# One buffer for the first weight matrix, and steps that run the second product ahead of the next first product, in an attention and two-layer mixture-of-experts kernel

## What is computed

```python
def _moe_ref(x, modality_id, w_gate, modality_bias, w1, w2):
    logits = x @ w_gate + modality_bias[modality_id]
    e_idx = np.argmax(logits, axis=1)
    ...
    for e in range(E):
        mask = e_idx == e
        if not mask.any():
            continue
        h = np.maximum(x[mask] @ w1[e], 0.0)
        out[mask] = gate_w[mask, None] * (h @ w2[e])

def _moe2_ref(x, w_gate, w_noise, noise, w1, w2):
    ...
    top2 = np.argpartition(-noisy_logits, 2, axis=1)[:, :2]
    for e in range(E):
        for k in range(2):
            mask = top2[:, k] == e
            h = np.maximum(x[mask] @ w1[e], 0.0)
            out[mask] += top2_w[mask, k, None] * (h @ w2[e])
```

## Time and profile before

| | us |
|---|---|
| median of three runs | 1207.27 |
| lowest and highest of them | 1205.92, 1213.23 |
| the profiled execution | 1211.57 |
| its span, first to last instruction | 1209.6 |

### The profile page before, as it was taken

How to read it: one execution, slowest core, us unless ns; L and a number is a source line. 1 busy time by engine, 2 the same in 40 slices (tenths; PEclk the granted TensorE clock), 3 DMA queues, 4 the chain that set the end, 5 groups by cost and what they waited for, 6 DMA issues and landing times.

```text
span 1209.6 us, 23517 instructions
## 1 busy us (share of the span) xinstructions
PE 964.3 (80%) x7285; PEld 922.6 (76%) x7286; DVE 541.7 (45%) x956; ACT 220.0 (18%) x393; POOL 361.1 (30%) x364
## 2 busy tenths in 40 slices
PE   6999998997989766627778687957887788979794
PEld 5888887997989765617778687957787778878793
DVE  8889978553223221476333324225224223343221
ACT  2223331121101011432012002102012021211010
POOL 6333341242212120054223314314313331241222
PEclk9999989898999987857899889979888888989898
DMA  6667820811101114404422414314313424221232
GB/s 245 209 219 243 290 80 18 320 41 35 48 28 55 29 41 131 156 2 157 132 35 42 139 28 131 54 29 111 72 32 77 99 39 132 34 48 28 33 46 39
DMA packets 54428, 112.70 MB, mean 93 GB/s; under 512 B 8592, under 2 KB 35472, under 8 KB 54288
## 3 DMA queue, kind: packets, MB, share of 16 engines
q1 hardware_dynamic: 34656, 71.07, 17.2%
q0 software_dynamic: 15744, 34.70, 14.5%
q10 hardware_dynamic: 3888, 4.89, 1.1%
HBM read 84.84 MB, written 25.81 MB: 91 GB/s over the span
## 4 chain that ended last, share of the span: by engine, by line
PE 73%; DVE 12%; issue 11%; DMA 2%; DVEq 1%; POOL 1%; ACT 0%; POOLq 0%; ACTq 0%
PE ps L1676 19%; PE ps L1677 18%; PE ps L1678 18%; PE ps L1588 2%; DVE hid_lo L1369 2%; PE ps L1548 2%; PE ps L1552 2%; PE ps L1517 2%; PE ps L1494 2%; PE ps L1579 1%; PE ps L1602 1%; DVE grow L890 1%; PE ps L1542 1%; PE ps L1613 1%; DVE x_lo L1364 1%
## 5 line engine op out<-in xcount | busy, mean ns | idle before, releaser
L1676 PE MATMUL ps<-x_hi,weights 128*128 128x256 f32 x984 | 300.2, 305 | 129.8 <-issue 119.2
L1676 PEld LDWEIGHTS ps<-x_hi,weights 128*128 128x128 f32 x984 | 201.4, 205 | 142.9 <-issue 136.3
L1678 PE MATMUL ps<-x_hi,weights 128*128 128x256 f32 x984 | 291.6, 296 | 1.7 <-issue 1.7
L1677 PE MATMUL ps<-x_lo,weights 128*128 128x256 f32 x984 | 291.8, 297 | 0.0
L1369 DVE SCALAR_TENSOR_TENSOR hid_lo<-ps,hid_hi 128x512 fp32r<-128x512 f32 x164 | 109.1, 685 | 347.4 <-ACT hid_hi L817 347.4
L817 ACT ACTIVATE hid_hi<-ps 128x512 fp32r<-128x512 f32 x164 | 93.7, 596 | 756.5 <-PE ps L1678 756.5
L1676 PE MATMUL ps<-weights,hid_hi 128*128 (+1 forms) x616 | 217.0, 352 | 10.4 <-issue 7.4
L669 POOL DMA_INDIRECT out_dram<-sy,dst_now x56 | 93.4, 1668 | 408.5 <-DVE sy L1382 270.7
L1677 PE MATMUL ps<-weights,hid_hi 128*128 (+1 forms) x616 | 212.2, 344 | 1.3 <-issue 1.3
L1678 PE MATMUL ps<-weights,hid_lo 128*128 (+1 forms) x616 | 211.3, 343 | 0.0
L1677 PEld LDWEIGHTS ps<-x_lo,weights 128*128 128x128 f32 x984 | 202.4, 206 | 0.0
(11 more groups left out here) (279 smaller groups left out, 1024.5 us busy)
## 6 DMA issues: line engine op xcount, KB each, us to landing
stage<-in_moe_w_dram SPq DMA_DIRECT2D x18, 1536.0 KB, 8.5
kv_in<-in_kv_T_dram SPq DMA_DIRECT2D x24, 512.0 KB, 5.7
kv_in<-in_kv_T_dram SPq DMA_DIRECT2D x24, 448.0 KB, 3.6
w_in<-in_w_T_dram SPq DMA_DIRECT2D x24, 258.5 KB, 4.1
out_dram<-zeros SPq DMA_DIRECT2D x25, 192.0 KB
x_rows<-y_tok ACTq DMA_DIRECT2D x24, 192.0 KB, 4.8
stage<-moe_rows SPq DMA_DIRECT2D x6, 768.0 KB, 4.8
stage<-in_moe_w_dram SPq DMA_DIRECT2D x2, 768.0 KB, 7.5
```

Source lines behind the costliest of these rows:

```text
L1676: pe.matmul(out_ps, hi, by_hi, start=first, stop=False)
L1677: pe.matmul(out_ps, hi, by_lo, start=False, stop=False)
L1678: return pe.matmul(out_ps, lo, by_hi, start=False, stop=final)
```

## The change

- `weights` has six parts instead of eight: one buffer for w1's two parts, two buffers for w2's. A tile `room` keeps the addresses of what follows.
- w1 of the next run is split in the last slot of a run (`w1_now`), once all four `up` of that slot are done; w2 of the next run is split in the first slot (`w2_now`). The loads of w1 and w2 wait for their own splits.
- A step on TensorE is now the whole second product of slot s (with a turn in its middle), then all four `up` of slot s+1, then a turn. There is one copy of it.
- The main loop's body holds two steps instead of four.
- On VectorE `hidden_low` comes in one group behind `result_copy`, and the second tile's `split_x` in the following step, between the two low halves of w1. In layer 1 the routing work is put between these in another way.
- `hidden_high` no longer waits for the second product; ScalarE splits weights at the start of a step and not between the hidden parts.

```diff
         W1_HI, W1_LO, W2_HI, W2_LO = (n * WSZ for n in range(4))
-        weights = sb("weights", [P, 2 * 4 * WSZ], F32R)
+        W2_STEP = 2 * WSZ
+        weights = sb("weights", [P, 6 * WSZ], F32R)
+        sb("room", [P, 2 * WSZ])
...
-        def pairs(eng, n, step, peel=0):
+        def pairs(eng, n, step, peel=0, inner=2):
...
                 def load_run(n, e):
-                    sp.wait_ge(s_lov[l], n * 3)
+                    sp.wait_ge(s_w2lo[l], n)
                     sp.nop(nofuse=True)
                     sp.wait_ge(s_lop[l], n)
                     sp.nop(nofuse=True)
-                    load_weights(l, e)
+                    load_w2(l, e)
+                    sp.wait_ge(s_w1lo[l], n * 2)
+                    sp.nop(nofuse=True)
+                    load_w1(l, e)
...
                     def work():
...
+                        if isinstance(s, int) and s == (ES - 1, 0)[l]:
+                            act.wait_ge(s_table[l], (2, 3)[l])
+                        if runs_from(l, s):
+                            run = lookup(act, slot_run[l], s, E - 1)
+                            with act.If(lookup(act, w1_now[l], s, 1) > 0):
+                                act.wait_ge(s_h[l], s * 4 + 4)
+                                act.nop(nofuse=True)
+                                for a in range(2):
+                                    split_w1(l, run + 1, a)
+                            with act.If(lookup(act, w2_now[l], s, 1) > 0):
+                                if not isinstance(s, int) or s > 0:
+                                    act.wait_ge(s_o[l], s * 2)
+                                    act.nop(nofuse=True)
+                                for a in (1, 0):
+                                    split_w2(l, run + 1, a)
...
+                        for q in range(4):
+                            hidden_high(s + 1, q)
...
+                dve.tensor_copy(w2_now[l][:, :], more[:, 0:n])
+                dve.tensor_copy(w1_now[l][:, 0:n - 1], starts[:, 1:n])
...
+                def hidden_rest(s, u):
+
+                    for q in range(3):
+                        hidden_low(s, q)
+                    split_x(s + 1, u, 0)
+                    hidden_low(s, 3)
...
+                        run = lookup(dve, slot_run[l], s, E - 1)
+                        change = lookup(dve, w1_now[l], s, 1)
+                        with dve.If(change > 0):
+                            low_w1(l, run + 1, 0)
+                        split_x(s + 1, 1 - u, 1)
+                        with dve.If(change > 0):
+                            low_w1(l, run + 1, 1)
+                        with dve.If(lookup(dve, w2_now[l], s, 1) > 0):
+                            low_w2(l, run + 1)
 
                     more(first)
                     result_copy(s, j, u)
-                    more(second)
+                    more(lambda: hidden_rest(s + 1, u))
...
-                    base = odd * 4 * WSZ + W1_HI
-                    pe.wait_ge(s_lov[l], 2 if isinstance(s, int) and s == 0 else run * 3 + 3)
+                    pe.wait_ge(s_w1lo[l], run * 2 + 2)
                     pe.wait_ge(s_sxc[l], s * TS + TS)
-                    if not isinstance(s, int) or s > 0:
-                        pe.wait_ge(s_hlo[l], (s - 1) * 4 + q + 1)
...
-                    if early(s + 1):
-                        whole(0)
-                    else:
-                        with pe.If(run_next % 2 < 1):
-                            whole(0)
-                        with pe.If(run_next % 2 > 0):
-                            whole(1)
+                    down_second(s, 0, run, two)
+                    down(s, 0, run, 0)
+                    slot_turn(l, s + 1, j + u, 1 - u, 1)
+                    down_second(s, 1, run, two)
+                    down(s, 1, run, 0)
+                    for q in range(4):
+                        up(s + 1, q, run_next)
+                    slot_turn(l, s + 2, j + 1, u, 0)
...
-                pairs(pe, SURE[l] - 2, slot_step, PEEL[l])
+                pairs(pe, SURE[l] - 2, slot_step, PEEL[l], 1)
```

More of the change, by code:

```diff
@@ L292, in attention_moe_moe @@
         s_w2 = [sem(f"s_w2{l}") for l in range(2)]
-        s_hi = [sem(f"s_hi{l}") for l in range(2)]
-        s_lov = [sem(f"s_lov{l}") for l in range(2)]
+        s_w1hi, s_w2hi = [sem(f"s_w1hi{l}") for l in range(2)], [sem(f"s_w2hi{l}") for l in range(2)]
+        s_w1lo, s_w2lo = [sem(f"s_w1lo{l}") for l in range(2)], [sem(f"s_w2lo{l}") for l in range(2)]
         s_lop = [sem(f"s_lop{l}") for l in range(2)]
@@ L326, in pairs @@
                 step(j, 1)
-            twos = (n // 2 - peel) // 2
+            twos = (n // 2 - peel) // inner
             with eng.Fori(0, twos) as q:
[L329 to L332, removed]
+                for d in range(inner):
+                    step(q * inner + (peel + d), 0)
+                    step(q * inner + (peel + d), 1)
+            for j in range(peel + inner * twos, n // 2):
                 step(j, 0)
@@ L835, in work @@
                     def work():
[L836 to L848 removed]
+                        if isinstance(s, int) and s == (ES - 1, 0)[l]:
+                            act.wait_ge(s_table[l], (2, 3)[l])
+                        if runs_from(l, s):
+                            run = lookup(act, slot_run[l], s, E - 1)
[10 more added lines that the diff above has]
+                                    split_w2(l, run + 1, a)
+                        elif s == 0:
+                            row_hot(0)
+                        for q in range(4):
+                            hidden_high(s + 1, q)
                     more(work)
                 if l == 1:
[L853 to L855 removed]
+                    for a in range(2):
+                        split_w1(1, 0, a)
+                    for a in (1, 0):
+                        split_w2(1, 0, a)
+                for q in range(4):
+                    hidden_high(0, q)
+                slots(act, l, step_slot, peel=PEEL[l])
         @block.vector
@@ L1338, in _ @@
                     full_slots(l)
-                def split_all(n, which=(1, 2, 3)):
-                    for q in which:
-                        split_piece(l, n, q)
-                def split_next(i):
-                    run = lookup(dve, slot_run[l], i, E - 1)
-                    with dve.If(lookup(dve, split_now[l], i, 1) > 0):
-                        split_all(run + 1)
                 def split_x(s, u, t):
```

217 lines of the change are left out of this document (69 added, 148 removed).

## The result

The changed kernel takes 1060.51 us (median of four runs, 1058.46 to 1063.83), the kernel before 1209.97 us in four runs of the same comparison. The ratio is 0.877, with a 95% interval from 0.873 to 0.881. The forecast was 1081 us in a range from 1050 to 1140. The profiled execution has a span of 1058.2 us, against 1209.6.

The account below looks back on a forecast made before the run. TensorE was taken as the bound (73% of the chain, "issue" 11%). The terms 1211.6 - 92 - 17 - 37 + 16 + 4 gave 1086 us for the profiled execution, 1081 us for the median, range 1050 to 1140 us.

Parts of the forecast that it names:

- Gaps between steps: TensorE's gaps at 38 step starts: the smaller body ends the long ones, 46 us instead of 137.8, so -92 us.
- What the gap is made of: TensorE's short gaps between steps: about three table reads less queued work, 0.7 to 2.0 us, taken as 1.2 us.
- Waits in a turn: TensorE's waits in turns for the rows' low part: 21.7 us falls to 5 us, so -17 us.
- Clock: TensorE's low clock behind long gaps: 15 of 52 us stay, so -37 us.
- Single buffer of w1: TensorE waits for w1's split behind five slots with one tile, 3.3 us each: +16 us.
- GpSimd beside VectorE: GpSimd's split slows VectorE's second-tile split in the first slot of 8 runs, 0.5 us each: +4 us.
- first rival: The main forecast with all terms as summed: 1081 us, between 1050 and 1105; chance 0.77.
- rival 3: TensorE's loops reload instructions at each of sixteen jumps back, 7 us each: 1192 us; chance 0.04.
- Rivals 2 and 5: 2: new serial chain takes part of gain, 1105-1140 us, chance 0.12; 5: hidden part 3 waits, 1240 us, 0.04.

Follow-up runs that it names:

- the run with one jump back: The changed kernel with eight steps instead of two in the body of layer 2's main loop, one copy: 1058.89 us, ratio 0.882.

## Why the prediction was right, point by point

**Gaps between steps: right.** The cause (a body that stays in the engine) and the size of what stays hold: 43.1 us in place of 137.8, forecast 46. Both figures hold two gaps in front of the last slots' second products (6.84 and 2.92 us before, 6.54 and 2.41 now), which I had taken for gaps between steps and which the change hardly touches. Without them a step's gap is (43.1 - 8.95) / 36 = 0.95 us, forecast 1.2. One step of the argument was incomplete. I put all of it on the body's size. The runs show two parts: size alone gives 60 us, and the single copy 43 us, by the tests that are gone (0.51 us a step, 19 us) and the first entries. I had counted the missing jumps as something, but without a price ("two jumps over parity copies are gone"). With the copies kept, a body that fits left "issue" at 61.2 us, so that the sum came out near is in part luck.

**What the gap is made of: right in kind.** I wrote that three reads less what is queued make the short gap. A read is 0.64 us. Three are 1.9 us, and moving two of them closes the gap, so what TensorE has queued covers some 1.4 us (an estimate, with the other register instructions left out): 0.5 us are left inside the body, and the jump back with its arithmetic adds 0.6.

**Waits in a turn: right, undersized.** I left 5 us, none is left. The four `up` of the next slot covered layer 1's routing work fully.

**Clock: right.** 38.5 us came back, forecast 37. The granted clock rose from 0.91 to 0.98 in layer 2. None of the gaps between steps up to 1.45 us lowered it; behind those of 1.8 us and more it fell in several places, as at the single read added. I had expected 1.2 GHz behind all five waits for w1; it came behind one, the longest.

**Single buffer of w1: the mechanism right, the term mis-sized.** Five waits, in slots with one tile, one in layer 1 and four in layer 2, as forecast. They took 10.9 us and not 16, for two reasons. For the case at 721.90 us: I gave VectorE's chain 8.8 us from the end of up 3 on, which the trace shows within 0.3 us, but I set TensorE's arrival at 6.0 us, and it came at 6.5 (1.31 us of gap, not 1.2, and the last matmul's full 0.34 us). That alone makes 2.8 into 2.4. The branch over the second tile, taken here, is 0.14 us of that gap. The sum then took 3.3, for which I had given no reason; the mean is 2.2.

**GpSimd beside VectorE: nothing of it.** `up` waits for the rows' low part in 2 places, 2.4 us in all. Both are at the first slot of a layer, and the kernel before has them too:

```profile
PE ps L1676 <- DVE x_lo L1364: 2.3, 2, 1.6
```

So the term, forecast 4 us, came to nothing.

**The sum.** The forecast missed 25 us of the span's 151: 6 in the gaps, 6 in the turns, 8 in the two costs, 2 in the clock, 2 in other stages, 1 in the pace. All misses had one sign. The median, 1060.5, lies in the first rival's own range. No gap over 3 us recurs (rival 3; the one of 6.54 us stands before layer 1's last slot), and its rule, a store with no gain for a loop, is refuted for these bodies: no packet of q8 between 600 and 940 us. Rivals 2 and 5 fall with the waits, 2.4 us for the split and 4.5 us for `hid_lo`.

## What to carry to other kernels

Count the instructions of a loop's body on each engine and look at the queue of instructions while it runs: if it moves packets, a taken jump to absent code was a gap of some 4 to 10 us on the engine that bounds, with a low clock behind it; straight code of the same length cost nothing. Look at the branch instructions by their lines: the stall is in their duration. Choosing a copy of the code by a test costs time even where all copies fit, here 0.5 us a step. A read of a table is 0.64 us on the reading engine: put it behind queued matmuls that don't need its value, which brought another 28 us here.

## What the runs showed of the hardware

- TensorE's bodies of 531, 618, 1,225, 1,235 and 1,238 instructions loop with hardly a packet on q8 (1 in 350 us for 1,225, 8 in 445 us for 1,235, none in 340 us for 618); with 2,448, 2,463 and 2,468 the queue moved packets while they ran.
- Fetched code that runs straight on keeps pace: 24 packets in 335 us, no gap but the one at the jump back, 5.04 us.
- An unconditional branch to the next instruction: no change of the gap (0.49 us against 0.50). A branch with a test, its target loaded: 0.07 us if not taken, 0.21 to 0.23 if taken, the same over 12 matmuls and over some 600 instructions. One taken to absent code: mostly 3.3 to 6.2 us; the idle time around it was 5.04 us in the run with one jump back, up to 10.2 us in others.
- A table read: 0.64 us where nothing covers it, of which the load is 0.30. A single one at a boundary is covered by what TensorE has queued.
- The granted level went to 1.2 GHz behind gaps of 1.8 us and more in some places, not in all: in the changed kernel after 2.53 us of idle time at 795.40 us the `up` matmuls start 0.21 us apart, after 2.37 us at 721.90 us they do not.

```profile
795.40 0.58 PE L1655 MATMUL ps<-x_hi,weights 128*128 128x256 f32 x1 [2.53 <-DVE weights L1086]
795.77 0.41 PE L1656 MATMUL ps<-x_lo,weights 128*128 128x256 f32 x1
795.99 0.41 PE L1657 MATMUL ps<-x_hi,weights 128*128 128x256 f32 x1
```
